# Attention and experts in one kernel: probability tiles turned in two steps by bank, a third probability buffer, nine value products, the threshold on ACT, a new order

## The chip, the cores and the metric

One NeuronCore of a Trainium2 chip runs the whole program. The metric is the device time of one execution in microseconds, the median of several runs. The engines are TensorE (PE, with its weight loads PEld), VectorE (DVE), ScalarE (ACT), GpSimd (POOL) and SyncE (SP, which issues DMAs). Each takes its instructions in order; semaphores tie them together.

## What is computed

Thresholded softmax attention over 4 batches, 8 heads, 576 positions and head size 64, and then a dense mixture of four experts on its output.

```
scores = q @ k.T / 8                      # per batch and head, 576 x 576
keep   = scores >= max(scores) - tau      # tau = 0.02
attn   = softmax of the kept scores (divided by sum + 1e-9)
x      = (attn @ v), heads side by side   # 2304 tokens x 512
p      = domain_probs / (sum + 1e-9)
out    = sum over e of p[:, e] * (relu(x @ w1[e]) @ w2[e])   # 512 -> 1024 -> 512
```

## The kernel before

TensorE multiplies in a fast format of reduced precision, so every operand is split in a high part (rounded copy, on ACT) and a low part (the rest, by a subtraction on DVE or POOL): q_hl, k_hh and k_ll, v_hl, pt_hi and pt_lo, x_hi and x_lo, w_hi and w_lo, h_hi and h_lo. Expert products are three matmuls (high by high, low by high, high by low).

Attention is cut in 144 units of 128 queries, in pairs of heads (28 pairs, 56 turns of one head each). A unit goes through: `s` (score products, PE, into s_ps or, for the first 27 units alternately, e_ps), `max` (negated row maximum, DVE), `thr` (maximum minus tau, POOL), `exp` (ACT, into p), `mask` (DVE: compare, multiply, row sum), `eps` (POOL), `rec` (reciprocal, DVE), `norm` (POOL, scales p in place), `tr` (five 128 x 128 transposes on PE into t_ps, two PSUM banks: four tiles in the first, the fifth in the second), `phi` (ACT, pt_hi from t_ps), `plo` (DVE, pt_lo from t_ps minus pt_hi). 576 keys fill four and a half tiles; the unused half of the fifth is zero in p and in v.

When the queries of a part (64 to 448 columns; 76 parts) are turned, `pv` makes ten products, five tiles by pt_hi and by pt_lo, into x_ps. The weights v_hl hold the high part of v in 64 columns and the low part in the other 64, so both halves of the output are added afterwards (`xo` on ACT, `xs` on DVE). After the last part of a pair, `x_hi` and `x_lo` split the result.

The experts work on four chunks of tokens (384, 640, 640, 640). The `up` products of a chunk need x_lo of all its pairs. Per expert there are `up` groups of 12 matmuls, followed by `hhi` (ACT, relu) and `hlo` (DVE), and `down` groups of 24 matmuls, followed by `acc` (DVE, weighted by prob). Groups alternate between the two banks of e_ps. The weight pieces go through `stage` (3 slots) by DMA, then `whi` (ACT) and `wlo` (POOL, every fourth on DVE at first) into a ring of 12.

The first 24 units (chunk 0) and three more run with no expert work beside them; the 117 others are spread between expert groups of the chunk before theirs. What stands where on each engine is decided before the program is built: `timeline` gives every step a due time from the tables ALONE and AMONG, and `settle` plays the steps out with assumed durations (TAKES); the order in which it starts them is each engine's order. Those are assumed durations, not measured times.

The waits that matter here: `exp(u)` writes p[u % 2] and waits for `tr(u - 2)` (L836); `tr(u)` waits for `norm(u)` and for `plo(u - 1)` (L747), since there is one t_ps; `s(u)` waits for `mask` of the unit that had its slot. At the start SP issues tau, q, k, dp, v (L627 to L654); POOL, ACT and PE wait for five memsets.

## Time and profile before

| | us |
|---|---|
| median of 3 runs | 1148.4 (1148.13 to 1151.02) |
| the profiled execution | 1148.03 |
| its span, first to last instruction | 1146.1 |
| PE busy | 1092.6 (95%) |
| POOL, DVE, ACT busy | 649.2, 603.0, 555.1 |
| mean granted clock of TensorE | 0.985 |

Busy time of PE overstates it: matmuls are pipelined, and one's printed duration is longer than the step from its start to the next one's. The step is what it costs on a full engine. Rows give the time of start in us from the span's start, the duration, the engine, the line, what is written and read, and in brackets the idle time before with what ended it. Rows by group give a line's instructions of one shape: busy us and mean ns of one, then the engine's idle time before them.

### The profile page before, as it was taken

The numbers are of one execution on the slowest core, as the hardware profiler recorded it, in microseconds if no ns is written. First come the engines' busy times: TensorE is split into PE (matmuls) and PEld (weight loads), VectorE is DVE, ScalarE is ACT, GpSimd is POOL, SyncE is SP. The second block draws the span as 40 slices with busy tenths as digits, with TensorE's granted clock in tenths as the row PEclk, the third lists the DMA queues.
The fourth block names the chain that finished last, engine by engine and source line by source line (L and its number), as shares of the span: only waits on it lengthen the run. The fifth ranks groups of instructions, "written<-read, shape, count | busy, mean of one in ns | idle before, by whom it ended". The sixth has DMA issues, their size and how long they took to land.

```text
span 1146.1 us, 18347 instructions
## 1 busy us (share of the span) xinstructions
PE 1092.6 (95%) x6536; PEld 1007.2 (88%) x6536; DVE 603.0 (53%) x1176; ACT 555.1 (48%) x1041; POOL 649.2 (57%) x823
## 2 busy tenths in 40 slices
PE   4766999999999999999999999999999999999998
PEld 3656998999899899998999989989899898989897
DVE  6887766778666465564653445756545321212121
ACT  5665656666666374462644635636445231414140
POOL 6865767776878385473754746728546142425250
PEclk9787999999999999999999999999999999999999
DMA  5331435343346143241333533304213132323221
GB/s 149 109 84 50 120 89 145 98 136 119 111 141 168 53 116 85 60 129 42 93 91 96 159 103 94 106 27 119 81 37 93 46 102 65 92 56 93 55 83 46
DMA packets 91801, 107.28 MB, mean 94 GB/s; under 512 B 43328, under 2 KB 47424, under 8 KB 91712
## 3 DMA queue, kind: packets, MB, share of 16 engines
q1 hardware_dynamic: 91712, 106.11, 33.0%
q8 instruction: 53, 0.87, 0.3%
q14 instruction: 36, 0.29, 0.1%
HBM read 101.36 MB, written 4.72 MB: 93 GB/s over the span
## 4 chain that ended last, share of the span: by engine, by line
PE 89%; DVE 5%; ACT 2%; issue 1%; POOL 1%; DMA 1%; SPq 0%; ACTq 0%; DVEq 0%
PE e_ps L801 11%; PE e_ps L803 11%; PE e_ps L802 11%; PE e_ps L787 11%; PE e_ps L788 11%; PE e_ps L789 11%; PE t_ps L750 6%; PE x_ps L762 4%; PE x_ps L761 4%; PE s_ps L740 3%; PE s_ps L741 3%; DVE pt_lo L924 1%; DVE neg_m L909 1%; DVE p L915 1%; DMA stage<-w 1%
## 5 line engine op out<-in xcount | busy, mean ns | idle before, releaser
L718 POOL TENSOR_TENSOR w_lo<-stage,w_hi 128x512 fp32r<-128x512 f32 x240 | 311.4, 1300 | 195.2 <-ACT w_hi L872 193.1
L787 PE MATMUL e_ps<-x_hi,w_hi 128*128 128x320 f32 (+1 forms) x896 | 285.7, 319 | 0.0
L789 PE MATMUL e_ps<-x_hi,w_lo 128*128 128x320 f32 (+1 forms) x896 | 280.6, 313 | 0.0
L788 PE MATMUL e_ps<-x_lo,w_hi 128*128 128x320 f32 (+1 forms) x896 | 280.5, 313 | 0.0
L801 PE MATMUL e_ps<-w_hi,h_hi 128*128 128x512 f32 x576 | 229.3, 398 | 0.0
L803 PE MATMUL e_ps<-w_hi,h_lo 128*128 128x512 f32 x576 | 225.5, 391 | 0.0
L802 PE MATMUL e_ps<-w_lo,h_hi 128*128 128x512 f32 x576 | 224.6, 390 | 0.0
L872 ACT ACTIVATE w_hi<-stage 128x512 fp32r<-128x512 f32 x256 | 158.0, 625 | 120.9 <-PE e_ps L803 93.7
L941 DVE SCALAR_TENSOR_TENSOR h_lo<-e_ps,h_hi 128x320 fp32r<-128x320 f32 (+1 forms) x224 | 111.7, 499 | 140.1 <-ACT h_hi L862 139.3
L787 PEld LDWEIGHTS e_ps<-x_hi,w_hi 128*128 128x128 f32 x896 | 168.9, 188 | 0.2
L788 PEld LDWEIGHTS e_ps<-x_lo,w_hi 128*128 128x128 f32 x896 | 168.8, 188 | 0.2
L789 PEld LDWEIGHTS e_ps<-x_hi,w_lo 128*128 128x128 f32 x896 | 168.5, 188 | 0.0
L862 ACT ACTIVATE h_hi<-e_ps 128x320 fp32r<-128x320 f32 (+1 forms) x224 | 99.4, 444 | 129.2 <-PE e_ps L789 128.8
L924 DVE TENSOR_TENSOR pt_lo<-t_ps,pt_hi 128x640 fp32r<-128x640 f32 x144 | 118.2, 821 | 46.0 <-ACT pt_hi L843 44.7
L915 DVE SCALAR_TENSOR_TENSOR p<-s_ps,thr,p 128x576 f32<-128x576 f32 x131 | 106.9, 816 | 62.8 <-ACT p L837 39.2
L843 ACT ACTIVATE pt_hi<-t_ps 128x640 fp32r<-128x640 f32 x144 | 101.1, 702 | 77.7 <-PE t_ps L750 74.9
L837 ACT ACTIVATE p<-s_ps,neg_m 128x576 f32<-128x576 f32 x131 | 96.6, 738 | 86.7 <-DVE neg_m L909 79.4
L750 PE MATMUL t_ps<-ident,p 128*128 128x128 f32 x720 | 108.9, 285 | 24.3 <-DVE pt_lo L924 22.6
L707 POOL TENSOR_SCALAR p<-p,inv 128x576 f32<-128x576 f32 x144 | 111.9, 777 | 35.3 <-DVE inv L920 35.2
L909 DVE TENSOR_REDUCE neg_m<-s_ps 128x1 f32<-128x576 f32 x131 | 98.6, 753 | 58.4 <-PE s_ps L741 57.5
L803 PEld LDWEIGHTS e_ps<-w_hi,h_lo 128*128 128x128 f32 x576 | 108.1, 188 | 24.0
L802 PEld LDWEIGHTS e_ps<-w_lo,h_hi 128*128 128x128 f32 x576 | 108.4, 188 | 19.7
(55 smaller groups left out, 1466.9 us busy)
## 6 DMA issues: line engine op xcount, KB each, us to landing
stage<-w SPq DMA_DIRECT2D x256, 256.0 KB, 2.8
k_raw<-kT SPq DMA_DIRECT2D x112, 144.0 KB, 2.9
v_raw<-v SPq DMA_DIRECT2D x56, 128.0 KB, 2.2
out<-acc SPq DMA_DIRECT2D x18, 256.0 KB, 2.0
q_raw<-qT SPq DMA_DIRECT2D x16, 144.0 KB, 2.9
q_raw<-qT SPq DMA_DIRECT2D x16, 128.0 KB, 2.7
q_raw<-qT SPq DMA_DIRECT2D x16, 112.0 KB, 2.6
q_raw<-qT SPq DMA_DIRECT2D x16, 96.0 KB, 2.5
```

The lines of the kernel that those rows point to most:

```text
L707: gp.tensor_scalar(p[u % 2][:, 0:SEQ], p[u % 2][:, 0:SEQ], col(inv, u), 1.0, ALU.mult, ALU.mult).then_inc(s_norm, 1)
L718: gp.tensor_tensor(w_lo[:, m % RING, :], stage[:, m % STAGES, :], w_hi[:, m % RING, :], ALU.subtract).then_inc(s_wl, 1)
L750: op = nc.tensor.transpose(t_ps[:, tile], p[u % 2][:, tile], ident[:])
L787: mm(ps[:, 0:n], w_hi[:, piece, tile], x_hi[:, k, cols], start=k == 0, stop=False)
L788: mm(ps[:, 0:n], w_hi[:, piece, tile], x_lo[:, k, cols], start=False, stop=False)
L789: op = mm(ps[:, 0:n], w_lo[:, piece, tile], x_hi[:, k, cols], start=False, stop=k == KT - 1)
L801: mm(ps, h_hi[:, f, tile], w_hi[:, piece, :], start=f == 0, stop=False)
L802: mm(ps, h_hi[:, f, tile], w_lo[:, piece, :], start=False, stop=False)
L803: op = mm(ps, h_lo[:, f, tile], w_hi[:, piece, :], start=False, stop=f == FT - 1)
L872: run(w_hi[:, m % RING, :], stage[:, m % STAGES, :], copy).then_inc(s_wh, 1)
L915: ve.scalar_tensor_tensor(out=tile, in0=s_slot(u), scalar=col(thr, u), in1=tile, op0=ALU.is_ge, op1=ALU.mult, accum_out=col(total, u)).the ...
L924: ve.tensor_tensor(pt_lo[:, :, pt_cols(u)], t_tile, pt_hi[:, :, pt_cols(u)], ALU.subtract).then_inc(s_plo, 1)
```

## The change

- `tr`, `phi` and `plo` of the first 27 units are done in two steps: the four tiles of the first bank, then the fifth tile. Each waits for the same step of the unit before. The other units keep one step, but their `plo` is two instructions as well.
- The last 64 keys stand twice in the fifth tile, on the key side of v (two loads of the tail in place of one and a memset) and in p (`norm` writes a scaled copy of the tail's 64 columns beside the tile, the twin, then the tile itself). `plo` subtracts in place in the upper 64 partitions of pt_hi's fifth tile, which then holds high parts below and low parts above. pt_lo has four tiles. `pv` makes nine products.
- Three buffers p; `exp(u)` waits for `tr(u - 3)`.
- `thr` is an ACTIVATE (Identity with scale and bias) on ACT in place of a tensor_scalar on POOL.
- At the start ACT issues the loads of k and dp, SP those of tau and q; a one-column Exp on ACT stands ahead of the first data. Two memsets for p and one for v_raw go, and ACT's and POOL's waits for the memsets and tau move or go. dp_sum and prob are a step of their own, no longer tied to the first `q_lo`.
- `timeline`, its tables and the durations in `settle` are new, so every engine has a new order.

```diff
-ALONE = dict(gap=2.19, turn=-3.03, start=-3.3, period=2.9, max=2.14, thr=0.91, exp=0.32, mask=0.33, eps=0.99,
+ALONE = dict(load=-5.59, q_hi=5.77, q_lo=4.84, k_hi=-2.03, k_lo=-10.84, v_hi=0.79, v_lo=-0.5, max=3.03, thr=5.27,
...
+def halves_of(u):
+    return (0, 1) if u < LONE else (2,)
+def turned(u, half=2):
+    return min(u, LONE) * 2 + max(u - LONE, 0) + (half + 1 if u < LONE and half < 2 else len(halves_of(u)))
...
-        p = [sb(f"p{i}", [P, PAD]) for i in range(2)]
+        p = [sb(f"p{i}", [P, PAD]) for i in range(P_BUFS)]
-        pt_lo = sb("pt_lo", [P, QT, PT_COLS], F32R)
+        pt_lo = sb("pt_lo", [P, QT - 1, PT_COLS], F32R)
+        TURNED = (slice(0, QT - 1), slice(QT - 1, QT), slice(0, QT))
...
-                    sp.dma_start(v_raw[0:TAIL, QT - 1, :], src[(QT - 1) * P:SEQ, :]).then_inc(s_v_ld, 16)
+                    for half in range(2):
+                        sp.dma_start(v_raw[half * TAIL:(half + 1) * TAIL, QT - 1, :], src[(QT - 1) * P:SEQ, :]
+                                     ).then_inc(s_v_ld, 16)
...
-                    gp.tensor_scalar(p[u % 2][:, 0:SEQ], p[u % 2][:, 0:SEQ], col(inv, u), 1.0, ALU.mult, ALU.mult
+                    gp.tensor_scalar(twin, tail, col(inv, u), 1.0, ALU.mult, ALU.mult).then_inc(s_twin, 1)
+                    pool.wait_ge(s_twin, u + 1)
+                    gp.tensor_scalar(tile, tile, col(inv, u), 1.0, ALU.mult, ALU.mult
                                      ).then_inc(s_norm, 1)
...
-                        pe.wait_ge(s_plo, u)
-                    for k in range(QT):
+                        pe.wait_ge(s_plo, turned(u - 1, half))
+                    for k in range(QT)[TURNED[half]]:
...
-                        mm(x_ps[:, bank, 0:part.n], tile, pt_hi[:, k, cols], start=k == 0, stop=False)
-                        op = mm(x_ps[:, bank, 0:part.n], tile, pt_lo[:, k, cols], start=False, stop=k == QT - 1)
+                        op = mm(x_ps[:, bank, 0:part.n], tile, pt_hi[:, k, cols], start=k == 0, stop=k == QT - 1)
+                        if k < QT - 1:
+                            mm(x_ps[:, bank, 0:part.n], tile, pt_lo[:, k, cols], start=False, stop=False)
...
+            for half in range(2):
+                nc.scalar.dma_start(k_raw[half * HD:(half + 1) * HD, :], kT[0]).then_inc(s_k_ld, 16)
+            nc.scalar.dma_start(dp_in[:], dp).then_inc(s_dp_ld, 16)
+            act.wait_ge(s_ident, 2)
+            run(warm[:], ident[:, 0:1], ACT.Exp)
...
+                    run(col(thr, u), col(neg_m, u), ACT.Identity, bias=tau_col[:, 2:3], scale=-1.0).then_inc(s_thr, 1)
...
-                    if u >= 2:
-                        act.wait_ge(s_tr, u - 1)
+                    if u >= P_BUFS:
+                        act.wait_ge(s_tr, turned(u - P_BUFS))
...
-                    ve.tensor_tensor(pt_lo[:, :, pt_cols(u)], t_tile, pt_hi[:, :, pt_cols(u)], ALU.subtract
-                                     ).then_inc(s_plo, 1)
+                    u, half = x
+                    dve.wait_ge(s_phi, turned(u, half))
+                    if half != 1:
+                        op = ve.tensor_tensor(pt_lo[:, :, pt_cols(u)], t_tile[:, 0:QT - 1, :],
+                                              pt_hi[:, 0:QT - 1, pt_cols(u)], ALU.subtract)
+                    if half != 0:
+                        lo = pt_hi[TAIL:P, QT - 1, pt_cols(u)]
+                        op = ve.tensor_tensor(lo, t_tile[TAIL:P, QT - 1, :], lo, ALU.subtract)
+                    op.then_inc(s_plo, 1)
```

How the order moves, at three places. First DVE at the start of the program, before:

```order
L886 TENSOR_TENSOR tau_col<-tau_col 128x1
L894 SCALAR_TENSOR_TENSOR q_hl0<-q_raw,tau_col,q_hl0 64x384
L898 TENSOR_REDUCE dp_sum<-dp_in 128x18
L900 TENSOR_SCALAR dp_sum<-dp_sum 128x18
L902 RECIPROCAL dp_sum<-dp_sum 128x18
L905 TENSOR_TENSOR prob<-dp_in,dp_sum 128x18 x4
L909 TENSOR_REDUCE neg_m<-s_ps 128x1
```

The same place on DVE after:

```order
L865 TENSOR_TENSOR tau_col<-tau_col 128x1
L877 TENSOR_REDUCE dp_sum<-dp_in 128x18
L879 TENSOR_SCALAR dp_sum<-dp_sum 128x18
L881 RECIPROCAL dp_sum<-dp_sum 128x18
L884 TENSOR_TENSOR prob<-dp_in,dp_sum 128x18 x4
L873 SCALAR_TENSOR_TENSOR q_hl0<-q_raw,tau_col,q_hl0 64x384
L888 TENSOR_REDUCE neg_m<-s_ps 128x1
```

The four steps on dp now stand ahead of the first low part of q (64x384, `q_lo`), for which the first score product waits.

Second, DVE in the middle of the first 24 units, before (p0 and p1 are the buffers of probabilities, written by `mask`; neg_m is `max`, inv is `rec`, 128x5x128 is `plo`):

```order
L924 TENSOR_TENSOR pt_lo<-t_ps,pt_hi 128x5x128
L915 SCALAR_TENSOR_TENSOR p0,total<-s_ps,thr,p0 128x576
L909 TENSOR_REDUCE neg_m<-e_ps 128x1
L920 RECIPROCAL inv<-total 128x1
L931 TENSOR_TENSOR x_sum<-x_ps,x_sum 64x384
L909 TENSOR_REDUCE neg_m<-s_ps 128x1
L924 TENSOR_TENSOR pt_lo<-t_ps,pt_hi 128x5x128
L915 SCALAR_TENSOR_TENSOR p1,total<-e_ps,thr,p1 128x576
```

The same engine after, in the same stretch (128x4x128 is the first step of `plo`, 64x128 its second):

```order
L904 TENSOR_TENSOR pt_lo<-t_ps,pt_hi 128x4x128
L888 TENSOR_REDUCE neg_m<-e_ps 128x1
L909 TENSOR_TENSOR pt_hi<-t_ps,pt_hi 64x128
L899 RECIPROCAL inv<-total 128x1
L894 SCALAR_TENSOR_TENSOR p1,total<-s_ps,thr,p1 128x576
L873 SCALAR_TENSOR_TENSOR q_hl1<-q_raw,tau_col,q_hl1 64x384
L904 TENSOR_TENSOR pt_lo<-t_ps,pt_hi 128x4x128
L894 SCALAR_TENSOR_TENSOR p2,total<-e_ps,thr,p2 128x576
L909 TENSOR_TENSOR pt_hi<-t_ps,pt_hi 64x128
```

`plo` is two rows with other work between them, and `mask` goes round three buffers.

Third, PE in the first 24 units, before, from one transposition to the value products (x_ps) behind the next:

```order
L750 MATMUL t_ps<-ident,p1 128x128 x5
L740 MATMUL s_ps<-k_hh0,q_hl0 128x288
L741 MATMUL s_ps<-k_ll0,q_hl0 128x288
L740 MATMUL s_ps<-k_hh0,q_hl0 128x288
L741 MATMUL s_ps<-k_ll0,q_hl0 128x288
L750 MATMUL t_ps<-ident,p0 128x128 x5
L761 MATMUL x_ps<-pt_hi,v_hl1 128x384
L762 MATMUL x_ps<-pt_lo,v_hl1 128x384
```

PE after, at such a place:

```order
L719 MATMUL t_ps<-ident,p2 128x128 x5
L709 MATMUL s_ps<-k_hh0,q_hl0 128x288
L710 MATMUL s_ps<-k_ll0,q_hl0 128x288
L709 MATMUL s_ps<-k_hh0,q_hl0 128x288
L710 MATMUL s_ps<-k_ll0,q_hl0 128x288
L719 MATMUL t_ps<-ident,p0 128x128 x4
L730 MATMUL x_ps<-pt_hi,v_hl0 128x384
L732 MATMUL x_ps<-pt_lo,v_hl0 128x384
...
L730 MATMUL x_ps<-pt_hi,v_hl0 128x384
L719 MATMUL t_ps<-ident,p0 128x128
```

The fifth tile can be turned behind other products than the four; the value products end on pt_hi alone.

## Rows read from the trace of the kernel before

**Rows 1.** Windows: us, then PE, PEld, DVE, ACT, POOL busy, clock, DMA share, GB/s.
```profile
8.50:113.90 105.40, 69.33 (x327) 61.21 (x328) 82.33 (x161) 62.17 (x108) 72.43 (x113) 0.85 0.35 97
113.90:1146.10 1032.20, 1023.29 (x6210) 946.00 (x6209) 518.04 (x1008) 489.81 (x930) 574.17 (x699) 1.00 0.33 93
```

**Rows 2.** Waits from 113.9 us on, the longest of PE: sum, times, longest.
```profile
PE t_ps L750 <- DVE pt_lo L924: 3.6, 2, 2.0
```

**Rows 3.** Groups by line and form, 8.5 to 113.9 us.
```profile
L750 PE MATMUL t_ps<-ident,p 128*128 128x128 f32 x130 | 25.1, 339 | 20.6 <-DVE pt_lo L924 18.9 <-POOL p L707 1.7
...
L924 DVE TENSOR_TENSOR pt_lo<-t_ps,pt_hi 128x640 fp32r<-128x640 f32 x25 | 20.5, 820 | 4.6 <-ACT pt_hi L843 4.4
...
L909 DVE TENSOR_REDUCE neg_m<-s_ps 128x1 f32<-128x576 f32 x15 | 11.3, 752 | 1.5 <-PE s_ps L741 1.3
...
L698 POOL TENSOR_SCALAR thr<-neg_m,tau_col 128x1 f32<-128x1 f32 x27 | 7.3, 270 | 5.5 <-DVE neg_m L909 5.2
```

**Rows 4.** Windows from the first row maximum on; the sum is over 10.5 to 113.9 us.
```profile
60.00:80.00 20.00, 12.59 (x75) 10.52 (x76) 17.98 (x36) 12.51 (x22) 13.60 (x25) 0.95 0.30 80
80.00:113.90 33.90, 23.27 (x112) 21.21 (x113) 24.11 (x50) 18.34 (x33) 18.45 (x33) 0.75 0.19 49
sum 103.40, PE 67.36 PEld 59.27 DVE 80.37 ACT 61.73 POOL 70.45; mean PE 16.84 PEld 14.82 DVE 20.09 ACT 15.43 POOL 17.61
```

**Rows 5.** Timeline of PE, value products: start, duration; two neighbours of each width.
```profile
200.20 0.37 PE L762 MATMUL x_ps<-pt_lo,v_hl 128*128 128x448 f32 x1
200.41 0.37 PE L761 MATMUL x_ps<-pt_hi,v_hl 128*128 128x448 f32 x1
...
217.52 0.27 PE L761 MATMUL x_ps<-pt_hi,v_hl 128*128 128x128 f32 x1
217.63 0.27 PE L762 MATMUL x_ps<-pt_lo,v_hl 128*128 128x128 f32 x1
...
403.02 0.28 PE L761 MATMUL x_ps<-pt_hi,v_hl 128*128 128x256 f32 x1
403.14 0.28 PE L762 MATMUL x_ps<-pt_lo,v_hl 128*128 128x256 f32 x1
```

**Rows 6.** Timeline of the start, 0 to 11 us.
```profile
3.73 0.58 SPq L644 DMA_DIRECT2D dp_in<-dp  x1
...
4.83 0.52 SPq L654 DMA_DIRECT2D v_raw<-v  x1
...
7.28 1.14 DVE L900 TENSOR_SCALAR dp_sum<-dp_sum 128x18 f32<-128x18 f32 x1
...
8.53 0.58 PE L740 MATMUL s_ps<-k_hh,q_hl 128*128 128x288 f32 x1 [8.53 <-POOL k_ll L689]
...
8.75 1.85 DVE L905 TENSOR_TENSOR prob<-dp_in,dp_sum 128x18 f32<-128x18 f32 x4
...
9.62 0.44 PE L740 MATMUL e_ps<-k_hh,q_hl 128*128 128x288 f32 x1
...
10.53 0.74 DVE L909 TENSOR_REDUCE neg_m<-s_ps 128x1 f32<-128x576 f32 x1
```

**Rows 7.** Groups by line and form, whole span: what sizes cost on each engine.
```profile
L707 POOL TENSOR_SCALAR p<-p,inv 128x576 f32<-128x576 f32 x144 | 111.9, 777 | 35.3 <-DVE inv L920 35.2
...
L843 ACT ACTIVATE pt_hi<-t_ps 128x640 fp32r<-128x640 f32 x144 | 101.1, 702 | 77.7 <-PE t_ps L750 74.9
...
L941 DVE SCALAR_TENSOR_TENSOR h_lo<-e_ps,h_hi 128x320 fp32r<-128x320 f32 x192 | 94.0, 490 | 137.1 <-ACT h_hi L862 136.6
...
L862 ACT ACTIVATE h_hi<-e_ps 128x320 fp32r<-128x320 f32 x192 | 83.7, 436 | 115.8 <-PE e_ps L789 115.7
...
L931 DVE TENSOR_TENSOR x_sum<-x_ps,x_sum 64x128 f32<-64x128 f32 x10 | 2.9, 288 | 5.2 <-ACT x_sum L849 5.0
L849 ACT ACTIVATE x_sum<-x_ps 64x128 f32<-64x128 f32 x10 | 2.7, 272 | 8.8 <-PE x_ps L762 8.5
...
L849 ACT ACTIVATE x_sum<-x_ps 64x64 f32<-64x64 f32 x8 | 1.8, 219 | 8.3 <-PE x_ps L762 8.2
```

282 lines of the change are left out of this document (121 added, 161 removed).

## The prediction

> **What bounds the kernel now.** I read the clocked windows first. From the first expert product at 113.9 us to the end, TensorE is busy 1023.3 of 1032.2 us [rows 1]; nothing else comes near (POOL 574, DVE 518, ACT 490). Of the 8.9 us without a matmul some lie at the very end (the last accumulation and store), and the longest named wait, a transpose held by pt_lo, sums to 3.6 us [rows 2]. So behind 113.9 us the time is the sum of TensorE's instructions, and only fewer or cheaper matmuls shorten it. Before 113.9 us it is different: TensorE is busy 69.3 of 105.4 us, DVE 82.3, POOL 72.4, ACT 62.2. No engine is full; 27 units of attention run with nothing to fill the gaps. TensorE idles 20.6 us ahead of transposes, 18.9 of them on pt_lo [rows 3]. DVE has the most work and sets the floor: from the first row maximum on it is busy 80.4 of 103.4 us (78%), but 90% between 60 and 80 us and 71% from 80 us to the first expert product [rows 4]. I call the part up to 113.9 us the head, the rest the main part. The profiled execution took 1148.03 us against a span of 1146.1, so 1.93 us lie around it; the median is 1148.4.
>
> **Part 1, the tenth value product.** Each of 76 parts makes five products with pt_hi and five with pt_lo now, nine afterwards: the last 64 keys stand twice in the columns of the fifth tile, the upper half holds the low parts, and one product takes both. Of the 76 parts, 68 run in the main part (counted in TensorE's order; 8 stand ahead of the first expert product in both kernels). What one product occupies is the step between two starts, not its printed duration: 0.11 us at 128 columns, 0.12 at 256, 0.20 at 448 [rows 5]. 192 columns lie between the first two (0.115), 64 columns cost what 128 do (0.11, the weight load sets it), 320 and 384 by the line between 256 and 448: 0.147 and 0.177. The sum over the main part: 8 of 64 and 10 of 128 columns 1.98, 14 of 192 1.61, 22 of 256 2.64, 6 of 320 0.88, 4 of 384 0.71, 4 of 448 0.82: **8.6 us less**, bare path, since the engine is full there. It could be 7.5 if 64 columns cost half. In the head the eight products lie beside other engines' work and count in part 3.
>
> **Part 2, the start.** k and dp are issued by ACT beside q on SP, and the activation table is loaded ahead of the data; before, dp was the fourth issue on SP's queue, at 3.73 us. In the new order the probabilities of the experts (dp_sum, prob) stand ahead of the first q_lo on DVE, where before they stood behind it. S(0), the first score product, waits for q_lo. Before: S(0) at 8.53, unit 1 behind it at 9.62, the DVE busy with prob from 8.75 on, and the first maximum only at 10.53 [rows 6]. Afterwards the first maximum no longer waits for prob, but S(0) does. Bounds: if the dp chain keeps its slow forms (the 18-column tensor_scalar took 1.14 us, four prob products 1.85), S(0) is late, near 9.2, and the maximum begins some 1.2 us behind it (unit 0's four products, 9.62 - 8.53, and the hand-over), at 10.4: gain 0.1. If dp lands early and nothing disturbs the chain, S(0) starts near 7 and the gain is 2.4. I take **0.9**, nearer to the slow row, because k_lo and v_lo of turn 0 run on POOL then too.
> The 1.14 us for 18 columns fell while POOL ran k_ll. The Trainium skill (GPSIMD Engine Reference, section 1, Specifications) says that POOL shares its SBUF interfaces with VectorE and contends with DVE instructions with two SBUF inputs or in a two-port mode. By that rule the chain is slow only where POOL is busy, and the start gains toward 2.4 if the chain is over before the first k_ll; the sum would then be 1.5 us lower. It does not change what I take.
>
> **Part 3, the rest of the head.** Transposes: for units below 27 the four tiles of the first PSUM bank and the one of the second are handed over apart, so tile 0 to 3 of the next unit can be turned while the fifth is still read. This splits phi and plo. DVE: the 640-column subtraction takes 0.82 [rows 3]; between 320 columns at 0.49 and 640 at 0.82 lie 0.69 for 512, and a 64-partition, 128-column piece takes 0.29 [rows 7]. That is 0.98, **+0.16 a unit**; 25 units before the first expert product make +4.0, and one more maximum stands there (+0.75): 80.4 becomes 85.2 us of DVE work. ACT: 640 columns 0.70; 512 by the line 0.60, plus 0.27 for 128: +0.17; the threshold comes over from POOL, priced by the smallest copy, 0.22 (between 0 and 0.27, what POOL takes for it). 27 times 0.39 is +10.5: ACT goes to about 73 of 97 us. Queued behind the threshold on ACT are exp or phi of another unit, which wait 0.22 longer; mask, its reader, no longer waits for POOL's queue. POOL: minus the threshold (0.27), plus the twin, a 64-column product between 0.27 (one column) and 0.78 (576 columns): 0.33, and a wait on it before the main one, about +0.1 a unit, +3 in all on 70. The extra v load is one more issue of 0.52 us a turn on SP [rows 6], 56 in 1146 us, 11 of them in the head; SP's queue is not the bound. SP's order moves loads by a step or two: no price.
> The third p buffer takes away exp's wait for the transposes two units back. The two-step turn shortens the loop through the first bank (turn, phi, plo, turn): phi and plo take 0.60 + 0.69 there instead of 0.70 + 0.82, and one transpose of five less stands in it. Both let DVE run fuller. How full is the open number. With 78% as before, 85.2 us of work last 109.2 us, 5.8 more than 103.4. With the 90% of 60 to 80 us they last 94.7, 8.7 less. With 95%, 89.7, 13.7 less. I take 88%, 96.8 us, **6.6 us less**: nearest to the window that shows what this code does when well interleaved, a little under because the last pair's chain (pv, xo, xs, x_hi, x_lo) leaves DVE gaps whatever the buffers.
>
> **Part 4, the main part otherwise.** Turning is not split there, but plo is (0.16 on DVE, 117 times, 19 us on 518 of 1032: hidden by its idle half). The threshold on ACT: 26 us on 490, hidden. The order is new everywhere. It has under 8.9 us of waits to win, and could add some; I put 0, from -4 to +6.
>
> **Sum.** 8.6 + 0.9 + 6.6 = 16.1: span 1130.0, with 1.93 around it **1131.9 us**, 1.4% under the median.
>
> **Rivals.**
> A, DVE eats the head's gain. For it: DVE is the fullest engine there, and the change gives it 4.8 us more. Against it: its idle time comes from waits that buffers and the split remove, and it reached 90% with two buffers. At 78 to 80% the head loses 3 to 6 us, the total gains 3.5 to 6.5: 1143, up to 1144.5.
> B, TensorE's clock. In the head it often runs at 1.2 GHz: unit 0's four products of 288 columns take 0.27 us each [rows 6], the granted clock averages 0.95 in 60 to 80 us and 0.75 after [rows 4], and its idle time there stands ahead of transposes [rows 3]. If the new order keeps it busy enough for 2.4 GHz throughout, the transposes and the value products on the chain shorten too and DVE nears 95%: head 14 us less, 1124.5. The Trainium skill (TensorE: Matmul & The Clock Gate, What's actually happening) says that idleness throttles and activity releases the clock, which is this rival's mechanism; the stretch with more waits has the lower clock, so the trace agrees so far.
> C, the other side: DVE or ACT hands expert banks back too late. Two e_ps banks alternate; a bank returns after h_hi (0.44) and h_lo (0.49) [rows 7], 0.93, while the other bank's group of 12 steps of 0.147 lasts 1.76. Slack 0.8. In the new order plo (0.98) or the threshold plus exp (0.96) can stand ahead of h_lo or h_hi. Where both hit one group, TensorE waits. Speaks for it: slack is less than one plo. Against it: with plo at 0.82 in the same queues the largest wait of TensorE in this stretch is another, and small [rows 2]. It decides from 16.1 / 224 = 0.07 us per group; at 0.1 each, 22 us, the time is 1154.
> D, the ninth product does not show: if weight loads, not products, paced TensorE in a way that the last product hid. The steps exclude it, as each product has its own load; 3%, 1140.
>
> **How the numbers follow.** Forecast (head 3 to 10 us less, main part 7 to 10 less) 0.70; B 0.09; A 0.11; C 0.05; D 0.03; others 0.02. The range for 8 in 10 takes the forecast and half of A and B: 1125 to 1141. A measurement of this kernel can tell about 0.3%, 3.4 us. Faster by more than that: the forecast, B, D, and most of A, 0.90. Within it: the rest of A and half of C, 0.06. Slower 0.04.
>
> **What would show it.** Right: the first expert product at 103 to 110 us; the L732 products number four a part, and from there to the end 1023 to 1025 us; pt_lo's waits ahead of transposes in the head cut to under 10 us; DVE at 86 to 90% there; first maximum at 9 to 10.4 us; the 4-tile subtraction near 0.69, the small one 0.29, the threshold 0.2 to 0.28. Wrong: waits of the expert products on h_lo in the main part (C), a second table load, DVE at 80% in the head (A), S(0) later than 9.3.

## The result, and the profile after

The changed kernel takes **1140.56 us**, median of 5 runs (1138.81 to 1141.61), beside 1150.35 (1148.13 to 1151.32) for the kernel before in the same comparison: a ratio of 0.992, 95% interval 0.9909 to 0.9932. Forecast were 1131.9. The sign is right and the time lies at the upper end of the range, but much of the gain is missing: 9.8 us came between the medians and 6.6 between the spans of the two profiled executions, where 16.1 were forecast. The profiled execution took 1141.22 us, its span 1139.5. The profiled execution of before lay below that kernel's median (1148.03) and this one's a little above its own, so the traces show less gain than the medians. Against the span of before, 1146.1, it splits like this:

| us | before | after | moved | forecast |
|---|---|---|---|---|
| first row maximum | 10.53 | 12.43 | +1.9 | -0.9 |
| from there to the first expert product (head) | 103.1 | 97.05 | -6.1 | -6.6 |
| from there to the end (main part) | 1032.5 | 1030.0 | -2.4 | -8.6 |

(Before, the first expert product starts at 113.64; the prediction put the border at 113.9.) The head came as forecast. The start and the main part did not.

Windows of the kernel after, columns as in [rows 1]: the head, then the main part, answering to [rows 1, 4].
```profile
12.43:109.48 97.05, 68.43 (x315) 57.34 (x314) 83.75 (x181) 69.55 (x160) 72.24 (x110) 0.84 0.38 102
109.48:1139.50 1030.02, 1016.60 (x6143) 938.28 (x6142) 548.41 (x1127) 512.43 (x1049) 575.49 (x699) 1.00 0.33 94
```
In the head DVE is busy 83.75 of 97.05 us, 86%. In the main part TensorE does the forecast work: 6143 matmuls where there were 6210, the tenth products less, and its busy time is 6.7 us shorter than in [rows 1]. But 13.4 us now hold no matmul; it was 8.9. So the 6.1 us that are missing in the main part are 4.5 of added idle time and 1.6 by which the fall of the busy time stayed short of the forecast 8.6.

Waits of PE, sum, times, longest. First one row of the head before, then after: five rows from 0 us to the first expert product, and all of the main part, answering to [rows 2, 3].
```profile
PE s_ps L740 <- DVE p L915: 9.9, 8, 2.2
...
PE s_ps L709 <- DVE q_hl L873: 11.1, 1, 11.1
PE t_ps L719 <- DVE pt_lo L904: 10.6, 10, 2.3
PE s_ps L709 <- DVE p L894: 4.8, 6, 1.7
PE t_ps L719 <- DVE pt_hi L909: 4.8, 8, 1.4
PE t_ps L719 <- POOL p L676: 3.7, 4, 1.6
...
PE s_ps L709 <- DVE p L894: 3.5, 5, 1.4
PE t_ps L719 <- POOL p L676: 3.1, 2, 2.2
PE x_ps L730 <- DVE pt_hi L909: 2.6, 2, 1.8
PE t_ps L719 <- DVE pt_hi L909: 1.3, 1, 1.3
PE e_ps L757 <- DVE h_lo L926: 0.9, 2, 0.6
```
In the head the waits of transposes on pt_lo fell from 18.9 to 10.6 us, and 4.8 on the small piece (L909, the second instruction of `plo`) stand beside them, so transposes wait 3.5 us less for `plo` as a whole. Score products wait 5.1 us less for the mask (DVE's p, 9.9 to 4.8). In the main part no row names pt_lo any more, but the two rows on pt_hi from DVE are waits on `plo` all the same, 3.9 us beside the 3.6 of [rows 2]. What was added is spread: score products wait for the mask, transposes for the scaling on POOL (its p), expert products for h_lo. The 1.3 us row is the wait that ends just at the border.

Groups of the main part after, by line and form: the sizes.
```profile
L904 DVE TENSOR_TENSOR pt_lo<-t_ps,pt_hi 128x512 fp32r<-128x512 f32 x119 | 81.9, 688 | 46.4 <-ACT pt_hi L822 45.2
L909 DVE TENSOR_TENSOR pt_hi<-t_ps,pt_hi 64x128 fp32r<-64x128 f32 x119 | 35.1, 295 | 1.6
L810 ACT ACTIVATE thr<-neg_m,tau_col 128x1 f32<-128x1 f32 x116 | 33.6, 289 | 75.8 <-DVE neg_m L888 75.3
L676 POOL TENSOR_SCALAR p<-p,inv 128x576 f32<-128x576 f32 x118 | 88.8, 752 | 11.0
L674 POOL TENSOR_SCALAR p<-p,inv 128x64 f32<-128x64 f32 x118 | 40.9, 346 | 24.6 <-DVE inv L899 24.6
```
The durations, 0.69, 0.30, 0.29 and 0.35 us, are near those of the prediction (0.69, 0.29, 0.22, 0.33); only the threshold is clearly longer, and it was free where it was tried alone. So what failed in the main part is hardly a duration. It is the word "hidden".

### The profile page after: what moved, and what is told of

It reads as the page before. It is cut to its first block, busy times and chain, and to the rows that moved or that the text cites. A ratio compares the mean times of both kernels' runs of the same rounds, so it can differ in the third digit from the quotient of the medians.

```text
span 1139.5 us, 18609 instructions
## 1 busy us (share of the span) xinstructions
PE 1086.4 (95%) x6460; PEld 997.0 (87%) x6460; DVE 637.0 (56%) x1320; ACT 585.6 (51%) x1213; POOL 652.0 (57%) x820
## 4 chain that ended last, share of the span: by engine, by line
PE 79%; DVE 6%; POOL 5%; DMA 4%; issue 2%; ACT 2%; SPq 1%; ACTq 0%; DVEq 0%
PE e_ps L773 11%; PE e_ps L771 11%; PE e_ps L772 11%; PE e_ps L757 10%; PE e_ps L759 10%; PE e_ps L758 10%; PE t_ps L719 6%; PE x_ps L730 3%; PE s_ps L709 3%; PE x_ps L732 3%; PE s_ps L710 3%; POOL w_lo L687 2%; DMA k_raw<-kT 2%; DVE q_hl L873 2%; DVE p L894 1%
## 5 line engine op out<-in xcount | busy, mean ns | idle before, releaser
L822 ACT ACTIVATE pt_hi<-t_ps 128x640 fp32r<-128x640 f32 (+2 forms) x171 | 105.3, 616 | 84.5 <-PE t_ps L719 81.0
L719 PE MATMUL t_ps<-ident,p 128*128 128x128 f32 x720 | 112.9, 285 | 22.6 <-DVE pt_lo L904 10.6
L904 DVE TENSOR_TENSOR pt_lo<-t_ps,pt_hi 128x512 fp32r<-128x512 f32 x144 | 99.0, 688 | 47.9 <-ACT pt_hi L822 46.3
L771 PEld LDWEIGHTS e_ps<-w_hi,h_hi 128*128 128x128 f32 x576 | 108.2, 188 | 19.6
L719 PEld LDWEIGHTS t_ps<-ident,p 128*128 128x128 f32 x720 | 89.5, 146 | 37.6 <-issue 17.8
```

What stands on the lines that cost most here:

```text
L719: op = nc.tensor.transpose(t_ps[:, tile], p[u % P_BUFS][:, tile], ident[:])
L771: mm(ps, h_hi[:, f, tile], w_hi[:, piece, :], start=f == 0, stop=False)
L822: run(pt_hi[:, TURNED[half], pt_cols(u)], t_tile[:, TURNED[half], :], copy).then_inc(s_phi, 1)
```

## The experiments

The part before the first expert product scatters: three kernels that keep before's order reached it at 111.98, 112.13 and 114.96 us. The main part scatters less: in four kernels whose main parts differ in one load at most it took 1030.0, 1031.5, 1030.5 and 1030.9. Medians scatter by 1 to 2 us too. The ratio to before, with its interval, is the better number. "Head" and "main" come from one profiled execution each, and that one can lie off the median: 1138.1 against 1141.4 us for nine products alone, 1151.6 against 1155.4 for all of the change in before's order, 1149.8 against 1146.3 without twin and small piece there, 1154.0 against 1149.8 for the changed kernel with the threshold on POOL. A difference of 2 or 3 us in these columns alone shows little.

| kernel | median | ratio, 95% | head | main |
|---|---|---|---|---|
| nine products alone | 1141.40 | 0.9933, 0.9917 to 0.9950 | 101.4 | 1024.2 |
| and threshold on ACT | 1140.86 | 0.9925, 0.9911 to 0.9939 | 104.4 | 1025.3 |
| and a third load of v | 1140.41 | 0.9927, 0.9912 to 0.9942 | 102.2 | 1027.3 |
| all of the change, before's order | 1155.44 | 1.0049, 1.0035 to 1.0064 | 102.6 | 1036.5 |
| same, two loads of v | 1152.87 | 1.0044, 1.0028 to 1.0059 | 107.8 | 1033.4 |
| same, threshold on POOL | 1156.75 | 1.0076, 1.0062 to 1.0089 | 105.3 | 1039.0 |
| same, no twin | 1147.73 | 0.9986, 0.9977 to 0.9996 | 103.4 | 1030.8 |
| same, no twin, no small piece | 1146.32 | 0.9974, 0.9962 to 0.9986 | 106.1 | 1031.1 |
| same, and two buffers | 1147.85 | 0.9984, 0.9972 to 0.9997 | 108.8 | 1027.1 |
| new order to the first expert product, before's behind | 1148.54 | 0.9998, 0.9989 to 1.0007 | 95.3 | 1038.9 |
| **the changed kernel** | 1140.56 | 0.9920, 0.9909 to 0.9932 | 97.1 | 1030.0 |
| changed, experts' probabilities later | 1141.13 | 0.9920, 0.9907 to 0.9933 | 99.4 | 1031.5 |
| changed, two loads of v | 1141.73 | 0.9932, 0.9920 to 0.9944 | 97.7 | 1030.5 |
| changed, banks handed over together | 1155.57 | 1.0061, 1.0048 to 1.0074 | 111.0 | 1030.9 |
| changed, threshold on POOL | 1149.75 | 1.0011, 0.9998 to 1.0023 | 100.9 | 1039.3 |
| changed, no twin | 1140.09 | 0.9923, 0.9909 to 0.9936 | 97.6 | 1029.5 |
| changed, no small piece | 1139.69 | 0.9914, 0.9899 to 0.9928 | 97.1 | 1029.1 |
| changed, neither | 1137.35 | 0.9898, 0.9885 to 0.9911 | 97.1 | 1027.7 |
| changed, more room at a chunk's end | 1150.84 | 1.0016, 1.0002 to 1.0029 | 96.7 | 1041.2 |

### The tenth product alone

```
-    mm(x_ps[:, bank, 0:part.n], tile, pt_hi[:, k, cols], start=k == 0, stop=False)
-    op = mm(x_ps[:, bank, 0:part.n], tile, pt_lo[:, k, cols], start=False, stop=k == QT - 1)
+    op = mm(x_ps[:, bank, 0:part.n], tile, pt_hi[:, k, cols], start=k == 0, stop=k == QT - 1)
+    if k < QT - 1:
+        mm(x_ps[:, bank, 0:part.n], tile, pt_lo[:, k, cols], start=False, stop=False)
```


> The kernel before with one thing left out: the tenth value product of each part, pt_lo of the fifth tile (so the low part of the last 64 probabilities is missing in the output). Order, buffers and all else are those of before. Theory (a value product costs its step on a full TensorE): from the first expert product to the end 8.6 us less than 1032.5, that is 1023 to 1025, and the head up to 1 us less: time 8.5 to 10 us under the kernel before. Rival (TensorE's gaps fill up: waits take the place of the products, as the engine reaches the next bank or transpose sooner): main part 2 to 6 us less, with new waits in it, time 3 to 6 us under before.

The main part fell by 8.2 us, where 8.6 were forecast; the ratio makes 0.67% or 7.7 us of the whole. No waits came in the products' place (8.5 us without a matmul, 8.9 before). Part 1 stands. And this edit alone takes as much off the time as the whole change, within the intervals, though it leaves out the low part of the last 64 keys, which the change keeps.

### Order against instructions

The planner of before was put into the changed kernel; then the two orders were joined at the first expert product:
```
-ORDER = settle(timeline())
+ORDER = old_order()                                  # all of before
+ORDER = joined(settle(timeline()), old_order())      # the other run: new head, before's main part
```


> All of the change (nine products, two-step turn, three p buffers, threshold on ACT, twin on POOL, loads at the start), but in the order of the kernel before: its tables, durations and rules decide; the two halves of tr, phi and plo stand side by side, and dp_sum and prob behind the first q_lo. Theory (the new waits of the main part, 13.4 us against 8.9, come from the new order): main part 1023 to 1026 us, no longer waits of transposes on norm than before; head 103 to 107 us from first maximum to first expert product, since the order sets how full DVE is: time 1136 to 1142. Rival (longer plo, the twin on POOL and the threshold on ACT make the waits, whatever the order): main part 1028 us or more, with waits on pt_hi and on norm as in the changed kernel, and time 1141 to 1146.

> The changed kernel with its own order up to the first expert product, and behind it the order of the kernel before on every engine. It differs from the changed kernel in the main part's order alone, and from the one with the old order throughout in the head's alone. Theory (the new main order costs what the ninth product gives): head as in the changed kernel, first expert product at 109 to 110 us; main part 1023 to 1026 instead of 1030.0; time 4 to 7 us under the changed kernel, 1134 to 1137. Rival (the new instructions make the waits): main part 1028 to 1031, time within 2 us of 1140.6.

I had blamed the new order for the waits. That theory fell in both runs: with the order of before and the new instructions the main part takes 1036.5 and 1038.9 us, 12 and 15 more than with nine products alone. The rival, that the new instructions make the waits, was right in kind, but both runs came out slower than it said. In an order not made for them the new instructions cost the time, and the new order wins half of it back in the main part.

### Which instruction, in the order of before

Threshold back on POOL:
```
-    act.wait_ge(s_max, u + 1)
-    run(col(thr, u), col(neg_m, u), ACT.Identity, bias=tau_col[:, 2:3], scale=-1.0).then_inc(s_thr, 1)
+    pool.wait_ge(s_max, u + 1)
+    gp.tensor_scalar(col(thr, u), col(neg_m, u), -1.0, tau_col[:, 2:3], ALU.mult, ALU.add).then_inc(s_thr, 1)
```


> The run before's order with all new instructions (its main part took 1036.5 us) with one of them undone: the threshold is again a tensor_scalar on POOL (0.34 us there), not an ACTIVATE on ACT (0.29 us). Theory (the chain from a unit's scores to its turned copy grew by about 0.80 us a unit: 0.29 for the threshold, which ACT now runs ahead of or behind the exponential that waits for the same maximum, 0.35 for the twin, 0.16 for the small piece, and the old order left no room for it): the threshold's share of the 12.3 us comes back, 12.3 x 0.29 / 0.80 = 4 to 5 us, main part 1031 to 1033 us, whole time 1149 to 1152 us. Rival one (ACT's queue alone pays: thresholds stand ahead of h_hi and w_hi work there): 10 to 12 us come back, main part 1024 to 1027, whole time 1143 to 1146. Rival two (POOL is the one that is overloaded by the twin): putting 0.34 us a unit more on POOL makes it worse, main part 1038 or more, whole time above 1156.

Twin and small piece left out behind the head:
```
+    if u < LONE:
         gp.tensor_scalar(twin, tail, col(inv, u), 1.0, ALU.mult, ALU.mult).then_inc(s_twin, 1)
         pool.wait_ge(s_twin, u + 1)
...
-    if half != 0:
+    if half == 1:
```


> The same order of before with all new instructions but two: in the units of the main part the twin of the last 64 keys on POOL and the small piece on DVE are left out (so the low part of the last tile is missing from the values there; the head keeps both). The threshold stays on ACT. Theory of the grown chain: 0.35 and 0.16 of 0.80 us come back, 7 to 8.5 us, main part 1028 to 1030 us, whole time 1146 to 1149 us. Rival one (ACT alone pays): nothing comes back, main part 1035 to 1038, whole time 1153 to 1157. Rival two (POOL's and DVE's load pays): all 12 us come back, main part 1024 to 1026, whole time 1142 to 1145.

Of the two, the first edit alone:

> The order of before with all new instructions (1155.4 us; without twin and small piece 1146.3), with the twin alone left out in the units of the main part. Theory (the small piece carries it here too, as it stands on DVE between pt_lo and the work that PE waits for; the twin makes the chain longer by 0.35 us where POOL has room): 2 to 4 of the 9 us come back, whole time 1151 to 1154 us. Rival (the twin carries it, POOL being the fullest engine after PE): 6 to 9 us come back, 1146 to 1149.5 us.

The threshold is not it: on ACT it is, if anything, better placed than on POOL, as that run's second rival said (above 1156 us). The twin is: without it the whole time falls by 7.7 us, and without the small piece too by 1.4 more, which is within the scatter. With both out the time, 1146.3 us, is the theory's. The theory of this last run (the small piece carries it) fell. What the small piece alone would give back in this order was not run. One 0.35 us instruction a unit on POOL, with the wait on it, costs 5.7 us in the main part, though POOL idles 44% of it. A twin placed behind the scaling, where it would add less ahead of the transposes, was not tried.

Waits of PE in the main part, order of before: with all instructions, then without the twin.
```profile
PE t_ps L1051 <- DVE pt_hi L1241: 4.4, 2, 2.3
PE s_ps L1041 <- DVE p L1226: 4.2, 4, 1.8
PE t_ps L1051 <- POOL p L1008: 1.4, 3, 0.6
...
PE t_ps L1052 <- DVE pt_hi L1242: 4.0, 2, 2.1
PE s_ps L1042 <- DVE p L1227: 4.0, 4, 2.1
PE t_ps L1052 <- POOL p L1009: 0.4, 2, 0.2
```
The direct wait on POOL shrinks by 1.0 us only. Of the 5.7 us, 2.9 are idle time of TensorE and 2.8 busy time (1020.8 against 1018.0 us); beyond the rows above I can't assign them.

Threshold on ACT as the only addition to nine products, then a third load of v, then the other way round: both tails by one DMA.
```
+    sp.dma_start(v_raw[TAIL:P, QT - 1, :], src[(QT - 1) * P:SEQ, :]).then_inc(s_v_ld, 16)
...
-    for half in range(2):
-        sp.dma_start(v_raw[half * TAIL:(half + 1) * TAIL, QT - 1, :], src[(QT - 1) * P:SEQ, :]).then_inc(s_v_ld, 16)
+    twice = src[(QT - 1) * P:SEQ, :].unsqueeze(0).to_broadcast([2, TAIL, HD])
+    sp.dma_start(v_raw[:, QT - 1, :], twice).then_inc(s_v_ld, 16)
```


> The kernel before, its own order, without the tenth product (as in the second experiment, whose main part took 1024.2 us and the whole 1141.4) and with one thing of the change alone: the threshold as an ACTIVATE on ACT in place of a tensor_scalar on POOL. The order was made for a threshold on POOL, and ACT now runs it directly ahead of the exponential of the same unit or where the list has it. Theory (each addition pays where the list has no room): 3 to 7 us more than the second experiment, main part 1027 to 1031, whole time 1144 to 1148 us; the same order with threshold on ACT and no twin and small piece took 1031.1 in its main part. Rival (the threshold on ACT is free, since POOL's 0.34 us goes; what that other kernel lost lies in the third buffer and in the head's new steps): within 1.5 us of the second experiment, main part 1023 to 1025.5, whole time 1140 to 1143 us.

> The opposite edit on the order of before: nine products, threshold on ACT (main part 1025.3, whole 1140.9), and one DMA more a turn that brings the last 64 rows of v into the second half of the tile too, where the probabilities are zero. No twin, no small piece, two buffers of p. Theory (the third issue on SP's queue costs): 3 to 6 us more, main part 1028 to 1031, whole time 1144 to 1147 us, with a wait of 1 us or more for k_ll or for p behind a late w piece. Rival (the issue is free; what separates this kernel from the one with third buffer, split steps and third DMA lies in the third buffer or the head): within 1.5 us, main part 1024.5 to 1026.5, whole time 1139.5 to 1142.5 us.

> The changed kernel, its own order, with the last 64 rows of v brought into both halves of the tile by one DMA instead of two (same bytes), so that SP's queue issues two DMAs a turn for v, as before the change, instead of three. Theory (the third issue, some 0.55 us of SP's queue in each of 56 turns, makes w and k pieces land late and ACT, whose queue stands in order, waits for them: its waits for w pieces rose from 25 to 38 us and for k from about nothing to 16): ACT's waits for DMA fall below 40 us together, main part 1026 to 1028.5, whole time 1136.5 to 1139 us. Rival (SP waits most of its time for free buffers anyway, so an issue more costs nothing, and the late pieces come from the new order of the loads): within 1.2 us of the changed kernel, 1139.3 to 1141.7 us.

> The order of before with all new instructions (main part 1036.5, whole 1155.4), with the last rows of v brought by one DMA instead of two. Theory: 3 to 6 us come back, main part 1031 to 1033.5, whole time 1149.5 to 1152.5 us, and the wait of 1.3 us for k_ll at 642 us is gone. Rival (the issue is free): main part 1035.5 to 1037.5, whole time 1154 to 1157 us.

By the whole time the threshold on ACT is free, as forecast, and so is the load: no ratio moved beyond its interval. The main part of the traces grew with each, by 1.1 and by 2.0 us, so a cost of 1 or 2 us there is not excluded. In the order of before one DMA for both tails took the main part from 1036.5 to 1033.4 us, as its theory said, and a wait of 1.3 us on k_ll went, but its time of 1152.9 lies between theory and rival and its ratio did not move. Last, two buffers instead of three (`P_BUFS = 2`):

> The order of before with the new instructions but without twin and small piece in the main part (1146.3 us), with two buffers of probabilities instead of three. What separates it still from nine products with the threshold on ACT (1140.9 us) are the third buffer, the steps split by bank in the head, the new start and the third load of v (free by its own run). Theory one (the third buffer costs, since exponentials run earlier and meet other work): 1141 to 1143.5 us. Theory two (the split steps of the head cost, in an order not made for them; the third buffer brings nothing in an order made for two): 1145 to 1148 us, and the head (first maximum to first expert product) stays at 103 to 107 us.

The third buffer neither costs nor clearly brings anything in that order: the head was 108.8 us instead of 106.1, the main part 1027.1 instead of 1031.1, and the ratios overlap. In the new order two buffers were not run. So the 5.5 us between 1146.3 and 1140.9 (nine products with the threshold on ACT) lie partly in a head whose split steps stand in an order not made for them (105.7 us on average in the six kernels with before's order and split steps, 102.8 in the four without split steps), and for the rest stay unexplained.

### The same in the new order

The same edits, made on the changed kernel: threshold on POOL, no twin, no small piece, neither.

> The changed kernel, its own order, with the threshold again on POOL instead of ACT; nothing else differs. Its main part took 1030.0 us and its head (first maximum to first expert product) 97.1. Theory of the grown chain: the main part falls by 1.5 to 3 us (to 1027 to 1028.5), while the head loses 0 to 3 us since POOL's 0.34 us and its queue stand ahead of the mask again; whole time 1138 to 1141 us. Rival one (ACT alone pays): main part 1024 to 1026, whole time 1134 to 1138. Rival two (POOL overloaded by the twin): main part 1031 to 1034, head 98 to 101, whole time 1143 to 1148.

> The changed kernel, its own order, with the twin (0.35 us on POOL ahead of the 0.75 us scaling) left out in the units of the main part, so that the low part of the last 64 keys is wrong there; the head keeps it. Theory of the grown chain: the waits of transposes on POOL (3.1 us in two places) and part of those behind them go, 2 to 4 us, main part 1026 to 1028 us, whole time 1136.5 to 1139 us. Rival one (ACT alone pays): within 1 us of the changed kernel, 1139.5 to 1141.5. Rival two (POOL's load pays for everything above the sum): main part 1024 to 1025, whole time 1134 to 1136.

> The changed kernel, its own order, with only the small piece on DVE (0.29 us, 64 partitions by 128 columns, right behind the 0.69 us subtraction) left out in the units of the main part, so that the low part of the last 64 keys is missing there; the twin stays. The prediction held it for hidden, since DVE idles half of the main part. Theory (it is not hidden: with the twin left out nothing much changed, with both left out 3.2 us came back, so the small piece alone is worth 2 to 3 us, through the pieces of work that wait right behind it): whole time 1137 to 1139 us. Rival (hidden as predicted; the 3.2 us were the two together, or scatter): 1139.8 to 1141.8 us.

> The changed kernel, its own order, with both the twin (0.35 us on POOL) and the small piece (0.29 us on DVE) left out in the units of the main part, so that the low part of the last 64 keys is wrong there. The twin alone gave back 0.5 us. Theory (the chain of the last units of a chunk of tokens ends late at the change of chunks, and each link counts there): main part 1025.5 to 1028.5 us, whole time 1136 to 1139. Rival (the new order was placed for these durations, its waits come from elsewhere, as from the maximum behind other work on DVE): main part 1028.5 to 1030.5, whole time 1139 to 1141.5.

The new order makes room for the twin: alone it is worth 0.5 us, the small piece alone 0.9, neither of which can be told from nothing. Both together are worth 3.2 (0.9920 against 0.9898, intervals barely overlapping). That a chain with either is still late where it matters is my reading, not shown. A threshold moved back to POOL costs 9 us here, where the theory had it gain up to 2.6 and the rival of a loaded POOL had it lose up to 7.4; probably because its place in the list was chosen for ACT's queue.

Timeline of the changed kernel at the change of one chunk of tokens to the next, 312 to 321 us.
```profile
312.59 0.71 PE L719 MATMUL t_ps<-ident,p 128*128 128x128 f32 x5
...
313.56 3.91 POOL L687 TENSOR_TENSOR w_lo<-stage,w_hi 128x512 fp32r<-128x512 f32 x3 [2.26 <-ACT w_hi L851]
...
315.23 0.29 DVE L909 TENSOR_TENSOR pt_hi<-t_ps,pt_hi 64x128 fp32r<-64x128 f32 x1
...
315.58 0.47 PE L730 MATMUL x_ps<-pt_hi,v_hl 128*128 128x448 f32 x1 [1.76 <-DVE pt_hi L909]
315.61 0.82 DVE L894 SCALAR_TENSOR_TENSOR p<-s_ps,thr,p 128x576 f32<-128x576 f32 x1
...
317.56 0.19 POOL L667 TENSOR_SCALAR total<-total 128x1 f32<-128x1 f32 x1
...
317.83 1.41 POOL L658 TENSOR_TENSOR k_ll<-k_raw,k_hh 128x576 fp32r<-128x576 f32 x1
...
319.21 0.32 POOL L674 TENSOR_SCALAR p<-p,inv 128x64 f32<-128x64 f32 x1
...
319.62 0.74 POOL L676 TENSOR_SCALAR p<-p,inv 128x576 f32<-128x576 f32 x1
...
320.42 0.77 PE L719 MATMUL t_ps<-ident,p 128*128 128x128 f32 x5 [2.23 <-POOL p L676]
```
These two waits, 1.76 and 2.23 us, 4.0 together, are the longest of the main part. The mask of the unit ends at 316.4. Its transposes start 4.0 us later, of which only 1.4 us are its own steps on POOL and DVE; nearly all of the rest is POOL's queue: three w_lo that piled up behind a late release of w_hi, and one k_ll. Without twin and small piece the two waits are still 1.45 and 2.11 us: most of them comes from the order, not from the new instructions.

The two waits cost more than their 4.0 us. The window right behind them (columns as in [rows 1]):
```profile
321.60:325.00 3.40, 3.40 (x15) 3.40 (x15) 2.25 (x5) 2.73 (x7) 3.40 (x5) 0.50 0.55 181
```
The granted clock is 0.50 there, the level of 1.2 GHz, and 1.00 on both sides of it. Expert products of 320 columns start every 0.27 us in it and every 0.15 us after it; twelve of them make an estimate of 1.4 us.

I tried to give such places room, with the units of a chunk placed 3 us earlier against its end (`end=15.6` for `end=12.6` in the planner):

> The changed kernel with one number of its planner changed: the attention units of a chunk are spread over the chunk's expert products less 15.6 us instead of less 12.6 us, so the last units of each chunk start some 3 us earlier against the change of chunks, and everything else is placed by the same rules. Theory (the two long waits near 315 and 320 us, 4.0 us together, are a lack of room ahead of the change of chunks): they shrink below 1.5 us together, main part 1025.5 to 1028.5, whole time 1136 to 1139. Rival (units that stand closer run into the queues of DVE and ACT elsewhere): the waits move, main part 1030 or more, whole time 1140 to 1148.

The waits moved and grew (6.2 us on POOL's p, 5.4 on the mask); the rival was right, and the time of 1150.8 is above even its range. No version found that keeps the low part of the last 64 keys clearly beats the changed kernel.

### The start and the head

The experts' probabilities put behind the fourth maximum on DVE, nothing else moved:
```
-ORDER = settle(timeline())
+ORDER = prob_after(settle(timeline()), "max", 3)
```

> The changed kernel with one step moved: dp_sum and prob stand on DVE behind the maximum of unit 3, not ahead of the first q_lo. Everything else keeps its place. Theory (the dp chain delays the first score product): the first score product starts near 8.0 us, when k_ll of turn 0 is written, instead of 11.10; the first maximum near 9.3 instead of 12.43; the chain's four steps then cost DVE 1 to 3.6 us later in the head, so the first expert product comes 1 to 3 us earlier than 109.5 and the time is 1138 to 1140. Rival (the loads of k, v and the first weight crowd each other, and the wait only hides that): the first score product at 10 us or later, time as the changed kernel, 1140.6. Second rival (DVE is so full in the head that a gain at its start is lost later): first maximum at 9.3, but the first expert product within 0.5 us of 109.5.

The start came out as it was meant to: first maximum at 9.43 instead of 12.43. But the first expert product started only 0.67 us earlier, and the whole did not change: less than the theory's 1 us, a little more than the second rival's 0.5. What the start wins is mostly swallowed in the head (99.4 us instead of 97.1).

Both steps of a unit's transposes wait for the whole unit before:
```
-    pe.wait_ge(s_plo, turned(u - 1, half))
+    pe.wait_ge(s_plo, turned(u - 1))
```


> The changed kernel, its own order, in which the two steps of a unit's transposes both wait for the whole of the unit before (both banks), not bank by bank; instructions and their order stay the same. Theory (the hand-over by bank is what shortens the head: first maximum to first expert product was 103.1 us before and is 97.1): 4 to 7 us of it are lost, head 101 to 104 us, whole time 1144.5 to 1148 us. Rival (the new order of the head brings it, not the hand-over by bank, since the fifth tile's piece follows the other by 0.3 us): head 97 to 99.5 us, whole time 1140.5 to 1143 us.

Windows of that kernel, head and main part, and its longest wait of PE in the head.
```profile
11.91:122.87 110.96, 69.69 (x314) 61.63 (x314) 84.22 (x181) 69.76 (x159) 71.81 (x111) 0.74 0.34 92
122.87:1153.80 1030.93, 1017.02 (x6145) 938.11 (x6143) 548.33 (x1126) 512.76 (x1048) 575.74 (x699) 1.00 0.33 94
```
```profile
PE t_ps L719 <- DVE pt_hi L909: 36.0, 21, 3.3
```
Same instructions, same order, one wait longer: the head takes 13.9 us more, about twice the 4 to 7 of the theory, and the main part is untouched. Transposes wait 36.0 us for the small piece where they waited 15.4 for both pieces. DVE's work is the same (84.2 us), only less dense: 76% instead of 86%. So the head's gain needs the hand-over by bank. It is not enough by itself: in the order of before, with the same hand-over, DVE was busy 85% of the head, but more of its work stood ahead of the first expert product (87.6 us), and the head took 102.6 us, 0.5 less than before. The 13.9 us are what the hand-over is worth in an order placed for it. TensorE's granted clock, 0.84 in the changed head, is 0.74 here, between its two levels of 1.2 and 2.4 GHz; it fell as its waits grew.

## Why the prediction was right or wrong

**Part 1, the tenth product: right.** 8.6 forecast, 8.2 measured alone, 68 instructions less. Rival D is out. (The "7.5 if 64 columns cost half" was mis-added: eight products at half of 0.11 us are 0.4 us, which makes 8.2.)

**Part 4, the main part otherwise: the step that failed.** It priced the split plo at "hidden by its idle half" and the order at 0. The bounds, -4 to +6, just miss what came: the main part should have taken 1032.5 - 8.6 = 1023.9 us and took 1030.0, 6.1 more. A third to a half of it (2.4 by the traces, 3.2 by the medians, at the edge of the noise) is the twin and the small piece, which ran on engines that idle about half of the time but stand in the chain mask, scaling, transposes, pt_lo, value product. The rest, 2.9 to 3.7 us, stays open. It is what is left over, not something that a run shows by itself: the new order's own waits, of which those at 315 and 320 us with the slow clock behind them are the largest seen, and perhaps 1 or 2 us of the third load, the threshold and the third buffer. The prediction priced the twin only in the head, at nothing in the main part, and argued "hidden" from an engine's share of busy time, not from the slack of the chain. In before's own order all additions together cost 12 us of main part, 5.7 of them the twin, and the prediction could not see this as it priced order and instructions each alone. The threshold on ACT was hidden in whole time, as said.

**Part 2, the start: wrong by 2.8 us, 0.7 of it seen at the end by its own run.** Timeline of the changed kernel's start, answering to [rows 6].
```profile
5.83 0.68 ACT L800 ACTIVATE k_hh<-k_raw 128x576 fp32r<-128x576 f32 x1 [1.61 <-DMA k_raw<-kT]
...
6.49 0.23 DVE L877 TENSOR_REDUCE dp_sum<-dp_in 128x18 f32<-128x72 f32 x1 [2.02 <-DMA dp_in<-dp]
6.59 1.40 POOL L658 TENSOR_TENSOR k_ll<-k_raw,k_hh 128x576 fp32r<-128x576 f32 x1 [5.11 <-ACT k_hh L800]
6.76 1.27 DVE L879 TENSOR_SCALAR dp_sum<-dp_sum 128x18 f32<-128x18 f32 x1
...
8.36 1.82 DVE L884 TENSOR_TENSOR prob<-dp_in,dp_sum 128x18 f32<-128x18 f32 x4
10.22 0.62 DVE L873 SCALAR_TENSOR_TENSOR q_hl<-q_raw,tau_col,q_hl 64x384 fp32r<-64x384 f32 x1
...
11.10 0.58 PE L709 MATMUL s_ps<-k_hh,q_hl 128*128 128x288 f32 x1 [11.10 <-DVE q_hl L873]
```
The chain was slow, as in the lower bound: 3.7 us from dp_sum to the end of prob. What I missed is when it starts: dp was issued early but landed only for 6.49. So q_lo, whose input was there at 7.0, ran at 10.22, and S(0) at 11.10 lies 1.9 behind the bound of 9.2; "S(0) later than 9.3" was one of the prediction's signs of being wrong. The other bound, S(0) near 7 and 2.4 us of gain, was out of reach too: with the chain moved away S(0) started at 8.09, behind k_ll (to 7.42) and q_lo (to 7.83), and the gain was 1.1.

The same edit settles what slows the 18-column instruction. Timeline of the run with the probabilities later.
```profile
6.02 1.40 POOL L667 TENSOR_TENSOR k_ll<-k_raw,k_hh 128x576 fp32r<-128x576 f32 x1 [4.53 <-ACT k_hh L809]
...
6.58 1.25 DVE L882 SCALAR_TENSOR_TENSOR q_hl<-q_raw,tau_col,q_hl 64x384 fp32r<-64x384 f32 x1 [2.52 <-ACT q_hl L803]
...
17.82 0.24 DVE L888 TENSOR_SCALAR dp_sum<-dp_sum 128x18 f32<-128x18 f32 x1
```
Away from k_ll the TENSOR_SCALAR takes 0.24 us, beside it 1.27. The q_lo that now meets k_ll takes 1.25 instead of 0.62; it reads two tiles in SBUF, so that agrees with the rule of the Trainium skill that the prediction weighed (GPSIMD Engine Reference, section 1, Specifications). The TENSOR_SCALAR reads one, so the rule covers it only in a two-port mode, and no run shows which mode it ran in.

**Part 3, the head: right in size, its mechanism shown in part.** 6.6 forecast, 6.1 measured. DVE's work came to 83.8 us (85.2 forecast) at 86% (88). The loop through the first bank is what it was held for: with the hand-over undone DVE falls to 76%, and the head takes 111.0 us, where the working gave 109.2 for 78%. But the prediction did not say that the order has to fit the hand-over (102.6 us in before's order), and what the third buffer adds in the new order no run shows, so part of the agreement in size is luck. The pt_lo waits came to 10.6 us, just above the 10 named, with 4.8 more on the small piece.

**The rivals.** A and B did not come: DVE kept 86%, and the granted clock of the head stayed at 0.84, as before (0.84 over 10.5 to 113.6 us). B's remark that the stretch with more waits had the lower clock is not borne out by the trace of before: TensorE's named waits are 8.6 of 20 us at 0.95 (60 to 80 us) and 11.3 of 33.6 at 0.75 (80 us to the first expert product), a smaller share. The run with the hand-over undone is the better witness. C has its place and not its size: expert products wait 0.9 us in all for h_lo. The case that came, gains in head and products with most of the latter eaten in the main part, was no rival at all. It stood only in the bounds of part 4.

## What to carry to other kernels

An instruction on an engine with idle time is hidden only if the chain it joins has slack where the full engine waits for that chain; look for these places (here the changes of chunks) one by one, not at shares of busy time. A hand-written or planned order is tuned to durations: price new instructions and the order together, and try the cheap part of a change alone first: here nine products alone, without what keeps the low part of the last keys, gave 0.67%, and the whole change 0.8%. Splitting a hand-over so that it follows the bank, not the unit, was worth 13.9 us in a stretch without filler work, in an order placed for it. In the order of before, with the same hand-over, the head was no shorter to speak of (102.6 to 108.8 us against 103.1).

## What the hardware showed that I had not expected

- Some VectorE instructions that start while POOL runs a two-input TENSOR_TENSOR are held until that one is over, however small they are: the 18 columns (1.27 us) end at 8.03, k_ll at 7.99; in the kernel with nine products at 8.45 and 8.41. The q_lo of 1.25 us ends 0.41 us behind its k_ll. In the whole changed kernel the w_lo that DVE makes from two tiles in SBUF takes 1.44 us (median of 5) when it starts beside such an instruction and 0.68 (median of 9) with none. Others are not held: the mask takes 0.82 us, pt_lo 0.69 and the small piece 0.30 in either case, all of which read one operand from PSUM; the reciprocal of a unit, with its one operand in SBUF, takes 0.16 in either case.
- One DMA issue on SP's queue can take three times its neighbours. All SP's w issues of 174 to 180 us in the run without twin and small piece in before's order (columns: least, median, most ns):
```profile
L969 SPq DMA_DIRECT2D stage<-w x3: 433/585/1754, 174.3 to 178.1; - x3
```
 The long one started at 176.28. But the piece that ACT then waited 2.2 us for was another: it was issued at 174.29 in 0.585 us and landed 4.9 us later, at 179.21, where the median of this kernel's transfers of w is 2.8. ACT's queue, which keeps its order, passed that on: a threshold behind the waiting w_hi held the mask of a unit, DVE idle for 3.42 us.
```profile
180.15 0.82 DVE L1227 SCALAR_TENSOR_TENSOR p<-s_ps,thr,p 128x576 f32<-128x576 f32 x1 [3.42 <-ACT thr L1143]
```
 What makes an issue or a landing slow stays open. A third load a turn is not needed for it: issues of w of 1.3 us and more stand in kernels with two loads of v too (1.34 and 1.51 with one DMA for both tails, 2.03 with nine products and the threshold on ACT).
